# First batch of an attention and feed-forward kernel: tile 1's scores in two PSUM banks of their own, the order of all engines for tiles 0 to 3 rewritten, two weight pieces requested at once

## The chip, the cores and the metric

The kernel runs on one NeuronCore of one Trainium2 chip. The metric is the device time of one execution in microseconds (us), as the median of several runs. A NeuronCore has five engines that run their own instruction streams and meet at semaphores: TensorE (PE, matrix products), VectorE (DVE), ScalarE (ACT), GpSimd (POOL) and SyncE (SP), which here only starts transfers. Sixteen DMA engines move the data for all of them.

## The reference, cut to what matters

Three stages follow each other. Stage one is attention in chunks of 32 queries; each chunk sees its own keys, 16 before, 8 after, and 8 memory keys. Stages two and three are feed-forward layers on its output.

```python
# q, k, v: (batch 4, heads 8, seq 768, dim 64); mem_k, mem_v: (4, 8, 8, 64)
for c in range(seq // 32):
    k_full = concat(mem_k, k[c_start - 16 : c_end + 8])      # clipped at both ends
    scores = (q_c @ k_full.T) / 8
    a = exp(scores - max(scores)); a = a / (sum(a) + 1e-9)
    out[c] = a @ v_full
x = out as (3072 tokens, 512)
h = x @ w_in                                    # 512 x 1024
solu = h * softmax(h)
x2 = (layernorm(solu) * g_ln) @ w_out           # 1024 x 512
h2 = x2 @ w2_in; g = h2 * clip(h2 + 3, 0, 6) / 6     # 512 x 2048
result = g @ w2_out                             # 2048 x 512
```

## The kernel before, in words

The kernel is written engine by engine, in one block with a function for each engine, and the orders of the instructions are written out by hand. Nothing reorders them: an engine that waits holds back everything behind it in its own list.

Attention goes in tiles of 96 queries. A batch has 8 tiles with all 8 heads of 96 queries each, and there are 4 batches. A tile n passes through these helpers:

- SP loads `q_in`, `k_in` and `v_in` (`load_q`, `load_k`, `load_v`; two buffers of each, by the tile's parity). The sources have rows of 64 floats, so that they move in pieces of 256 bytes. A window of keys takes four transfers, and a fifth for the memory keys in tiles 0 and 1. `load_q(0, t)` waits until the query tile two before has been transposed, `load_k(0, t)` likewise for keys. All of these transfers leave on SP's queue (q1 in the rows); for tile 0 part of the keys leaves on ACT's (q10).
- PE transposes them into PSUM (`turn_q`, `turn_k`, L991), ACT copies them out (`copy_q`, `copy_k`), PE makes the scores (`scores`, L1044), in 48 small products.
- DVE takes the maximum of half the heads (`max_half`, L1786), ACT the exponentials of that half (`exp_half`, L1497), DVE the sum and its reciprocal (`den_half`, `rec_half`) and the scaling (`scale_half`, L1806).
- PE transposes the probabilities by halves (`turn_half`, L1052), ACT copies them (`copy_half`, L1472), PE makes the weighted sum of values (`attend`, L1073), and ACT and DVE split it into a high and a low part (`high_x`, `low_x`), which is the input x of the next stage.

In a call such as `exp_half(1, 0)` the first number is the tile and the second the half. Stage two works on 128 tokens at a time. `hidden_part(m, x)` (L1114) is a quarter of h for token block m, six products of 512 columns. Block 0 needs x of tiles 0 and 1 (`x_lo_done` 2), and of `w_in` it needs the split pieces 0 and 1 in part 0 and pieces 2 and 3 in part 1 (`w_lo_done` 2 and 4). After part 3 come `max_hidden`, `exp_hidden` (L1512), `solu_of` (L1853), the statistics, and the normalisation on POOL.

The weights come in eight pieces of 512 KB, four of `w_in` and four of `w_out`. POOL requests each (`load_weights`, on the software queue q0) and casts it to its high part (`high_weights`); DVE makes the low part of the first four (`low_weights`, L1771). The first request waits for the first query tile.

Only in the first batch is all of this written out (`first_batch` of each engine), because the pipeline fills there: PE has no products of stage two to do yet. `keep_busy(n)` gives PE n products of 128 by 128 whose result nobody reads. From the second batch on, a regular pattern (`batch`) runs with PE's products back to back. Tile n's scores are in PSUM banks 0 and 1, for every n, so that `scores(n)` waits for the exponentials of tile n-1.

Of the kernel before, what the change touches and what calls it, by code (L numbers as in the profile page):

```python
# [11 lines left out]
P = 128  # L12
# [6 lines left out]
def attention_solu_hardswish(  # L19
# [69 lines left out]
    with ExitStack() as ctx:  # L89
# [80 lines left out]
        score_ps = banks[0:TQ, 0:2, :].rearrange("p b (h n) -> p (b h) n", n=NK)  # L170
        turn_ps = [banks[:, 2, :], banks[:, 3, :]]
# [190 lines left out]

        def is_ahead(n):
            return n >= NA - AHEAD
# [94 lines left out]
        def _(sp):  # L459
# [228 lines left out]
        def _(pool):  # L688
# [60 lines left out]
            pool.wait_ge(fixed_ready, HALF_READY)  # L749
            pool.wait_ge(q_in_here[0], 16)  # L750

            def first_batch():
                load_weights(0)
                high_weights(0)
                load_weights(1)
# [3 lines left out]
                load_gain()  # L759
# [227 lines left out]
        def _(pe):  # L987
# [39 lines left out]
            def scores(n, very_first):  # L1027
# [7 lines left out]
                if very_first:  # L1035
                    pe.wait_ge(score_cleared, 2)
                else:
                    pe.wait_ge(sexp_done, 2 * n)
                for x in range(HB):
                    for c in range(TQ // CHUNK):  # L1040
                        rows = slice(CHUNK * c, CHUNK * (c + 1))
                        for e in range(2):
                            r = slice(D * e, D * e + D)
                            mm = pe.matmul(chunk_cols(score_ps[rows, HB * e + x, :], c), q_of[r, x, rows],  # L1044
# [126 lines left out]
            def keep_busy(times):  # L1171


                for _ in range(times):
                    pe.matmul(banks[:, 7, 0:P], ident[:, :], ident[:, :], start=True, stop=True)

            def first_batch():
                pe.wait_ge(fixed_ready, IDENT_READY)
                keep_busy(8)
# [4 lines left out]
                scores(0, True)  # L1184
# [12 lines left out]
                scores(2, False)  # L1197
# [3 lines left out]
                keep_busy(4)  # L1201
# [3 lines left out]
                keep_busy(2)  # L1205
                pe.wait_ge(prob_copied, 2)
                turn_half(1, 1)
                keep_busy(2)
# [21 lines left out]
                scores(4, False)  # L1230
# [15 lines left out]
                scores(5, False)  # L1246
# [25 lines left out]
                scores(6, False)  # L1272
# [21 lines left out]
                scores(7, False)  # L1294
# [11 lines left out]
            def batch(b, last=False, start=0):  # L1306
                for kk in range(start, TILES):
# [16 lines left out]
                    if w["own"]:  # L1324
                        scores(n, False)
# [113 lines left out]
        def _(act):  # L1439
# [50 lines left out]
            def exp_half(n, half):  # L1490
# [5 lines left out]
                for h in range(HB * half, HB * (half + 1)):  # L1496
                    last = nc.scalar.activation(prob[n % 2][:, h, :], score_ps[:, h, :], ACT.Exp, bias=smax[:, h:h + 1],  # L1497
# [70 lines left out]
            def first_batch():  # L1568
# [200 lines left out]
        def _(dve):  # L1769
# [3 lines left out]
            def clear_scores():  # L1773
                for half in range(2):
                    nc.vector.memset(score_ps[:, HB * half:HB * (half + 1), :], MASKED).then_inc(score_cleared, 1)

            def max_half(n, half):
# [8 lines left out]
                nc.vector.tensor_reduce(smax[:, hs], score_ps[:, hs, :], AX_X, ALU.max, negate=True  # L1786
# [121 lines left out]
            def first_batch():  # L1908
# [4 lines left out]
                max_half(1, 0)  # L1913
                den_half(0, 1)
                scale_half(0, 0)
                rec_half(0, 1)
                max_half(1, 1)
                scale_half(0, 1)
                den_half(1, 0)
                rec_half(1, 0)  # L1920
                low_weights(0)
                scale_half(1, 0)
                den_half(1, 1)
                rec_half(1, 1)
                max_half(2, 0)
                scale_half(1, 1)
                low_weights(1)
                max_half(2, 1)
                low_x(0, 0, 0)
                den_half(2, 0)  # L1930
                rec_half(2, 0)
                low_weights(2)
                scale_half(2, 0)
                low_x(1, 1, 0)
                low_weights(3)
                den_half(2, 1)
                max_half(3, 0)
                rec_half(2, 1)
                scale_half(2, 1)
                max_half(3, 1)  # L1940
# [270 lines left out]
```

## Time and profile before

| | us |
|---|---|
| median of 3 runs | 904.52 (903.02 to 905.22) |
| the profiled execution's own time | 903.32 |
| its span, from the first instruction to the last | 901.5 |
| PE busy | 876.4 |
| DVE busy | 646.7 |
| ACT busy | 460.5 |
| POOL busy | 263.8 |

The span is what the profile's clock covers, and the execution's own time holds 1.8 us around it. Engines overlap, so that busy times don't add up. All of the change lies in about the first 40 us of the span.

### The profile page before, as it was taken

To read this page: it belongs to the slowest core of one execution; us is meant where nothing else is said; L and a number is where in the kernel's file an instruction comes from. 1 tells how busy PE (TensorE), PEld (TensorE's weight loads), DVE (VectorE), ACT (ScalarE), POOL (GpSimd) and SP (SyncE) were. 2 spreads that over 40 slices of the span, in tenths; PEclk is the share of its full clock that TensorE was granted. 3 is DMA by queue.
4 is the path that set the end of the run, shared out by engine and by line. 5 is a ranking of instruction groups with operands and counts; after the bars stand their busy time and mean duration, and the time that the engine had idled before them with its cause. 6 is when DMAs were issued, how large, how long until landed. Compare 5 with 4: busy or idle time off the path is not lost.

```text
span 901.5 us, 18748 instructions
## 1 busy us (share of the span) xinstructions
PE 876.4 (97%) x7170; PEld 792.1 (88%) x7170; DVE 646.7 (72%) x1054; ACT 460.5 (51%) x1129; POOL 263.8 (29%) x308
## 2 busy tenths in 40 slices
PE   6899999999999999999999999999999999999998
PEld 5778988898888989899888888888799999999998
DVE  4768768787666778857685545554898887979784
ACT  5667555656565554537674555545754333333331
POOL 2474355465241453550122333223510000000000
PEclk8999999999999999999999999999999999999999
DMA  9965265554644474477733333333996434354341
GB/s 194 192 147 159 73 181 162 178 173 135 176 131 133 121 231 149 155 262 286 268 114 138 129 118 129 136 140 109 352 371 237 151 102 157 96 162 140 118 141 47
DMA packets 143496, 148.56 MB, mean 165 GB/s; under 512 B 91194, under 2 KB 102970, under 8 KB 142394
## 3 DMA queue, kind: packets, MB, share of 16 engines
q1 hardware_dynamic: 130272, 102.12, 37.3%
q0 software_dynamic: 7920, 38.94, 12.5%
q10 hardware_dynamic: 5226, 6.44, 2.2%
q8 instruction: 52, 0.85, 0.4%
q14 instruction: 26, 0.21, 0.1%
HBM read 89.92 MB, written 57.54 MB: 164 GB/s over the span
## 4 chain that ended last, share of the span: by engine, by line
PE 83%; DMA 5%; DVE 5%; ACT 3%; POOL 2%; issue 1%; SPq 1%; ACTq 0%; POOLq 0%; DVEq 0%
PE banks L1408 25%; PE banks L1147 25%; PE banks L1099 20%; PE banks L1114 3%; PE banks L1073 3%; PE banks L1044 2%; PE banks L991 2%; PE banks L1052 2%; PE banks L1090 2%; ACT prob L1497 1%; DMA xs_raw<-x_scratch 1%; POOL x_mix L897 1%; DMA x_mix<-x_scratch 1%; DMA x_mix_scratch<-x_mix 1%; DVE prob L1806 1%
## 5 line engine op out<-in xcount | busy, mean ns | idle before, releaser
L1408 PE MATMUL banks<-vs,gs 128*128 128x256 f32 x2016 | 242.8, 283 | 0.9 <-DMA vs<-v_split_scratch 0.8
L1408 PEld LDWEIGHTS banks<-vs,gs 128*128 128x128 f32 x2016 | 242.2, 192 | 1.6 <-DVE gs L1771 1.1
L1147 PE MATMUL banks<-xs,ws 128*128 128x512 f32 x1008 | 230.6, 390 | 0.5 <-ACT part L1550 0.2
L1147 PEld LDWEIGHTS banks<-xs,ws 128*128 128x128 f32 x1008 | 188.2, 188 | 41.6 <-issue 1.9
L1728 ACT CAST gs<-gs_raw 128x1792 fp32r<-128x1792 f32 x48 | 81.4, 1697 | 124.0 <-DVE gs_raw L2104 124.0
L1099 PE MATMUL banks<-y_t,w_out 128*128 128x384 f32 x768 | 141.1, 338 | 0.0
L1099 PEld LDWEIGHTS banks<-y_t,w_out 128*128 128x128 f32 x768 | 133.1, 188 | 0.8
L1099 PE MATMUL banks<-w_in,x_t 128*128 128x512 f32 x480 | 114.8, 395 | 1.1 <-DVE solu L1853 1.1
L1099 PEld LDWEIGHTS banks<-w_in,x_t 128*128 128x128 f32 x480 | 88.7, 188 | 19.9 <-DVE solu L1853 1.3
L2104 DVE TENSOR_TENSOR gs_raw<-gs_raw 128x256 f32<-128x256 f32 x192 | 82.2, 429 | 31.8 <-DMA gs_raw<-g_scratch 26.7
L1771 DVE TENSOR_TENSOR gs<-gs_raw,gs 128x1792 fp32r<-128x1792 f32 (+2 forms) x50 | 97.5, 1953 | 0.0
L1566 ACT ACTIVATE relu<-part,small 128x512 f32<-128x512 f32 x72 | 52.2, 724 | 86.1 <-DVE part L1895 86.0
L1497 ACT ACTIVATE prob<-banks,small 96x128 f32<-96x128 f32 x256 | 89.6, 370 | 9.3 <-DVE small L1786 9.3
L1904 DVE SCALAR_TENSOR_TENSOR part<-relu,part 128x512 f32<-128x512 f32 x72 | 53.7, 745 | 44.4 <-ACT relu L1566 44.4
L1895 DVE TENSOR_TENSOR part<-part,banks 128x512 f32<-128x512 f32 x72 | 49.4, 686 | 43.4 <-PE banks L1147 43.1
L1806 DVE TENSOR_TENSOR prob<-prob,small 96x512 f32<-96x512 f32 x64 | 56.3, 879 | 1.9
L941 POOL TENSOR_TENSOR ws<-ws_raw,ws 128x256 fp32r<-128x256 f32 x42 | 34.6, 835 | 74.1 <-ACT ws L1529 74.1
L1472 ACT COPY prob_t<-banks 128x384 f32<-128x384 f32 x64 | 28.3, 482 | 53.3 <-PE banks L1052 49.4
L1497 ACT ACTIVATION_READ_ACCUMULATOR prob<-banks,small 96x1 f32 x256 | 53.6, 209 | 0.0
L1839 DVE TENSOR_REDUCE small<-banks 128x1 f32<-128x1024 f32 x24 | 29.3, 1221 | 26.2 <-PE banks L1099 18.0
L1550 ACT COPY part<-banks 128x512 f32<-128x512 f32 x72 | 41.7, 579 | 12.1 <-PE banks L1147 11.0
L1786 DVE TENSOR_REDUCE small<-banks 96x4 f32<-96x512 f32 x64 | 42.1, 681 | 7.6 <-PE banks L1044 6.4
(104 smaller groups left out, 1012.7 us busy)
## 6 DMA issues: line engine op xcount, KB each, us to landing
g_scratch<-part SPq DMA_DIRECT2D x96, 256.0 KB, 2.0
gs_raw<-g_scratch SPq DMA_DIRECT2D x45, 512.0 KB, 4.0
x_scratch<-x_out ACTq DMA_DIRECT2D x32, 192.0 KB, 3.8
out_dram<-o_stage SPq DMA_DIRECT2D x11, 512.0 KB, 5.7
q_in<-in_q_dram SPq DMA_DIRECT2D x28, 192.0 KB, 3.0
v_split_scratch<-v_split POOLq DMA_DIRECT2D x3, 1792.0 KB, 7.6
ws<-w_split_scratch SPq DMA_DIRECT2D x21, 256.0 KB, 6.2
vs<-v_split_scratch SPq DMA_DIRECT2D x3, 1792.0 KB, 10.2
```

The source lines that it names most:

```text
L1099: mm = pe.matmul(psum, stationary(a, kc), moving(m, kc), start=(x == 0), stop=(x == len(passes) - 1))
L1147: mm = pe.matmul(ps, ws[:, W_OF[i], a, kc, :], xs[g][X_OF[i]][:, m, kc, :], start=(fresh and x == 0), stop=(x == len(passes) - 1), skip_gr ...
L1408: mm = pe.matmul(m_ps[i][:, s, :], gs[x][:, a, G_OF[i], s * P:(s + 1) * P], vs[p][:, m, V_OF[i], :], start=(p == 0 and s == 0 and y == 0), ...
L1497: last = nc.scalar.activation(prob[n % 2][:, h, :], score_ps[:, h, :], ACT.Exp, bias=smax[:, h:h + 1], accum_out=ssum[:, h:h + 1])
L1566: nc.scalar.activation(relu[r][:, :], src, ACT.Relu, bias=three).then_inc(relu_done[kind], 1)
L1728: nc.scalar.copy(gs[n % NGS][:, HI, :, :], gs_raw[n % NGS][:, :, :]).then_inc(gs_hi_done, 1)
L1771: return nc.vector.tensor_tensor(dst, src, hi.bitcast(F32), ALU.subtract)
L1786: nc.vector.tensor_reduce(smax[:, hs], score_ps[:, hs, :], AX_X, ALU.max, negate=True).then_inc(smax_done, 1)
L1806: nc.vector.tensor_tensor(prob[n % 2][:, hs, :], prob[n % 2][:, hs, :], srec[:, hs].unsqueeze(2).broadcast_to([TQ, HB, NK]), ALU.mult).the ...
L1895: nc.vector.tensor_tensor(part[e][:, :], part[e][:, :], ps, ALU.add).then_inc(sum_done[kind], 1)
L1904: nc.vector.scalar_tensor_tensor(out=part[e][:, :], in0=relu[r][:, :], scalar=6.0, in1=acc_ps[g] if kind == 21 else part[e][:, :], op0=ALU ...
L2104: nc.vector.tensor_tensor(gs_raw[x][:, to, :], gs_raw[x][:, a, :], gs_raw[x][:, b, :], op).then_inc(gt_done, 1)
```

## The change

Tile 1's scores get PSUM banks 6 and 7 (`second_score_ps`), cleared at the start by two more memsets on DVE. `scores(1)` then waits for that clearing, and no longer for the exponentials of tile 0; `scores(2)` waits for tile 0's exponentials alone. The fillers of `keep_busy` write to other banks. POOL no longer waits for the first query tile, requests g_ln first and then weight pieces 0 and 1 one behind the other. SP requests the values of tiles 0 and 1 ahead of queries and keys of tile 3. The lists of PE, ACT and DVE are put in another order for tiles 0 to 3.

```diff
@@ SP, first_batch
                 load_k(0, 2)
+                load_v(0, 0)
+                load_v(0, 1)
                 load_q(0, 3)
                 load_k(0, 3)
-                load_v(0, 0)
-                load_v(0, 1)
                 load_q(0, 4)
@@ POOL
-            pool.wait_ge(fixed_ready, HALF_READY)
-            pool.wait_ge(q_in_here[0], 16)
             def first_batch():
+                load_gain()
                 load_weights(0)
+                load_weights(1)
                 high_weights(0)
-                load_weights(1)
                 load_weights(2)
                 high_weights(1)
                 load_weights(3)
-                load_gain()
                 high_weights(2)
@@ PE, scores
-                if very_first:
-                    pe.wait_ge(score_cleared, 2)
+                if n < 2:
+                    pe.wait_ge(score_cleared, 2 * n + 2)
                 else:
-                    pe.wait_ge(sexp_done, 2 * n)
+                    pe.wait_ge(sexp_done, 2 if n == 2 else 2 * n)
@@ PE, first_batch
                 pe.wait_ge(qk_copied, 2)
                 turn_k(1, early_ps[1])
-                keep_busy(4)
-                scores(1, False)
+                keep_busy(4, 3)
                 pe.wait_ge(qk_copied, 3)
                 turn_q(2, early_ps[0])
-                keep_busy(2)
+                scores(1)
                 pe.wait_ge(qk_copied, 4)
                 turn_k(2, early_ps[1])
+                keep_busy(6, 3)
                 turn_half(0, 0)
                 pe.wait_ge(qk_copied, 5)
                 turn_q(3, early_ps[0])
-                scores(2, False)
+                scores(2)
                 turn_half(0, 1)
                 pe.wait_ge(qk_copied, 6)
                 turn_k(3, early_ps[1])
-                keep_busy(4)
+                pe.wait_ge(sexp_done, 4)
+                keep_busy(4, 7)
                 pe.wait_ge(prob_copied, 1)
                 turn_half(1, 0)
                 attend(0, 0, True)
...
                 attend(0, 1, False)
-                keep_busy(3)
-                scores(3, False)
-                pe.wait_ge(prob_copied, 3)
-                turn_half(2, 0)
+                keep_busy(3, 7)
                 pe.wait_ge(qk_copied, 7)
                 hidden_part(0, 0)
                 hidden_part(0, 1)
+                pe.wait_ge(prob_copied, 3)
+                turn_half(2, 0)
                 pe.wait_ge(qk_copied, 8)
+                scores(3)
                 hidden_part(0, 2)
@@ ACT, first_batch
                 exp_half(0, 1)
+                act.wait_ge(scores_done, 4)
                 copy_q(2, early_ps)
                 copy_k(2, early_ps)
                 exp_half(1, 0)
+                copy_half(0, 0)
                 exp_half(1, 1)
-                copy_half(0, 0)
                 copy_half(0, 1)
                 act.wait_ge(scores_done, 6)
                 copy_q(3, early_ps)
                 act.wait_ge(av_done, 1)
                 copy_half(1, 0)
+                high_x(0, 0, 0)
                 copy_k(3, early_ps)
-                high_x(0, 0, 0)
+                copy_half(1, 1)
                 exp_half(2, 0)
-                copy_half(1, 1)
+                high_x(1, 1, 0)
                 exp_half(2, 1)
-                high_x(1, 1, 0)
                 copy_half(2, 0)
+                copy_half(2, 1)
                 exp_half(3, 0)
-                copy_half(2, 1)
```

SP's list, from `load_q(0, 3)` on, before. `q_in` is a query tile, `k_in` a window of keys in four transfers, `v_in` values; the six transfers of `v_in` are tile 0's.

```order
L475 DMA q_in<-in_q_dram 96x8x64
L422 DMA k_in<-in_k_dram 56x8x64
L422 DMA k_in<-in_k_dram 8x8x64
L422 DMA k_in<-in_k_dram 24x8x64
L422 DMA k_in<-in_k_dram 32x8x64
L422 DMA v_in<-in_v_dram 40x8x64
L422 DMA v_in<-in_v_dram 8x8x64
L422 DMA v_in<-in_v_dram 24x8x64
L422 DMA v_in<-in_v_dram 32x8x64
L426 DMA v_in<-in_mem_v_dram 8x8x64
L429 DMA v_in<-in_v_dram 16x8x64
```

SP's list of the change, from the last transfer of tile 0's values to the last of tile 3's keys.

```order
L433 DMA v_in<-in_v_dram 16x8x64
L426 DMA v_in<-in_v_dram 56x8x64
L426 DMA v_in<-in_v_dram 8x8x64
L426 DMA v_in<-in_v_dram 24x8x64
L426 DMA v_in<-in_v_dram 32x8x64
L430 DMA v_in<-in_mem_v_dram 8x8x64
L479 DMA q_in<-in_q_dram 96x8x64
L426 DMA k_in<-in_k_dram 56x8x64
L426 DMA k_in<-in_k_dram 8x8x64
L426 DMA k_in<-in_k_dram 24x8x64
L426 DMA k_in<-in_k_dram 32x8x64
```

Tile 3's queries and keys moved behind the eleven transfers of both value tiles; the last transfer of its keys stands where the last one of tile 1's values stood, the 30th of SP's list.

DVE's list before, from `low_weights(1)` to the first half of tile 2 scaled and after it. `w_in` rows are `low_weights`, `x_t` rows `low_x` of tiles 0 and 1, L1796 and L1801 `den_half` and `rec_half`.

```order
L1771 TENSOR_TENSOR w_in<-w_first,w_in 128x1024
L1786 TENSOR_REDUCE small<-banks 96x4
L1771 TENSOR_TENSOR x_t<-banks,x_t 128x4x96
L1796 TENSOR_SCALAR small<-small 96x4
L1801 RECIPROCAL small<-small 96x4
L1771 TENSOR_TENSOR w_in<-w_later,w_in 128x1024
L1806 TENSOR_TENSOR prob_60<-prob_60,small 96x512
L1771 TENSOR_TENSOR x_t<-banks,x_t 128x4x96
L1771 TENSOR_TENSOR w_in<-w_later,w_in 128x1024
```

DVE's list of the change over the same work.

```order
L1791 TENSOR_REDUCE small<-banks 96x4
L1775 TENSOR_TENSOR x_t<-banks,x_t 128x4x96
L1775 TENSOR_TENSOR w_in<-w_first,w_in 128x1024
L1775 TENSOR_TENSOR x_t<-banks,x_t 128x4x96
L1775 TENSOR_TENSOR w_in<-w_later,w_in 128x1024
L1801 TENSOR_SCALAR small<-small 96x4
L1806 RECIPROCAL small<-small 96x4
L1811 TENSOR_TENSOR prob_60<-prob_60,small 96x512
L1775 TENSOR_TENSOR w_in<-w_later,w_in 128x1024
```

The second `x_t` row (`low_x` of tile 1) moved ahead of `low_weights(2)` and of the scaling of tile 2, and `low_weights(1)` moved behind the first `x_t` row. Between the second `x_t` row and the last `w_in` row (`low_weights(3)`) there was nothing, and now there are four instructions.

## Rows read from the trace of the kernel before

**Rows 1.** The page: busy time, and the engines' shares of the last chain.

```profile
PE 876.4 (97%) x7170; PEld 792.1 (88%) x7170; DVE 646.7 (72%) x1054; ACT 460.5 (51%) x1129; POOL 263.8 (29%) x308
...
PE 83%; DMA 5%; DVE 5%; ACT 3%; POOL 2%; issue 1%; SPq 1%; ACTq 0%; POOLq 0%; DVEq 0%
```

**Rows 2.** Chain that ended last, first 43 us: start, us, what.

```profile
9.72 2.78 ACT prob L1497 x16
...
16.74 2.89 ACT prob L1497 x16
...
21.69 0.85 PE banks L991 x4
...
23.96 0.83 PE banks L1073 x16
...
26.05 1.51 ACT prob L1497 x8
...
29.76 0.67 PE banks L1044 x46
...
30.91 4.16 PE banks L1114 x18
...
38.11 1.21 ACT h_exp L1512 x2
```

**Rows 3.** Timeline of SP's queue: start, us, what was issued.

```profile
9.37 2.33 SPq L422 DMA_DIRECT2D k_in<-in_k_dram  x4
...
14.23 5.97 SPq L422 DMA_DIRECT2D v_in<-in_v_dram  x4
20.24 0.63 SPq L426 DMA_DIRECT2D v_in<-in_mem_v_dram  x1
20.92 0.32 SPq L475 DMA_DIRECT2D q_in<-in_q_dram  x1
24.25 0.32 SPq L497 DMA_DIRECT2D q_raw<-in_q_dram  x1
```

**Rows 4.** Tile q_in, 0 to 40 us: time from issue to landing.

```profile
DMA to landing us min/median/max: 3.0/4.9/5.9
```

**Rows 5.** Stretches: busy us (count) by engine, clock, DMA share, GB/s.

```profile
10.00:15.00 5.00, 2.37 (x55) 2.22 (x56) 1.78 (x6) 2.90 (x16) 2.05 (x3) 0.76 1.19 181
15.00:20.00 5.00, 2.12 (x30) 1.96 (x34) 3.14 (x8) 3.82 (x19) 2.42 (x3) 0.84 0.98 225
20.00:25.00 5.00, 5.00 (x86) 4.60 (x75) 4.47 (x7) 1.05 (x3) 2.08 (x2) 0.72 1.00 189
```

**Rows 6.** DMA queues, 10.74 to 22.35 us: packets, MB, share of 16 engines.

```profile
q1 hardware_dynamic: 3956, 0.96, 56.4%
q0 software_dynamic: 420, 1.49, 48.2%
```

**Rows 7.** Timeline of PE, ACT and DVE, to 48 us: start, us, instruction.

```profile
19.77 1.09 PE L1044 MATMUL banks<-k_t,q_t 64*32 64x64 f32 x48 [2.88 <-ACT prob L1497]
...
21.49 1.06 PE L991 MATMUL banks<-ident,k_in 128*128 128x128 f32 x4
...
24.82 0.48 ACT L1472 COPY prob_t<-banks 128x384 f32<-128x384 f32 x1 [2.22 <-PE banks L1073]
25.20 0.59 ACT L1447 COPY k_t<-banks 128x512 f32<-128x512 f32 x1
...
29.17 0.51 ACT L1507 CAST x_t<-banks 128x384 fp32r<-128x384 f32 x1
29.71 0.56 DVE L1771 TENSOR_TENSOR x_t<-banks,x_t 128x384 fp32r<-128x384 f32 x1
30.19 1.22 DVE L1771 TENSOR_TENSOR w_in<-w_later,w_in 128x1024 fp32r<-128x1024 f32 x1
...
40.23 1.27 DVE L1853 SCALAR_TENSOR_TENSOR solu<-h_exp,small,banks 128x1024 f32<-128x1024 f32 x1
...
47.66 0.60 PE L991 MATMUL banks<-ident,k_in 128*128 128x128 f32 x4
```

More of the change, by code:

```diff
@@ L170, in attention_solu_hardswish @@
         score_ps = banks[0:TQ, 0:2, :].rearrange("p b (h n) -> p (b h) n", n=NK)
+        second_score_ps = banks[0:TQ, 6:8, :].rearrange("p b (h n) -> p (b h) n", n=NK)
         turn_ps = [banks[:, 2, :], banks[:, 3, :]]
@@ L360, in attention_solu_hardswish, with scores_of @@
         IDENT_READY, THREE_READY, HALF_READY = 2, 3, 4
+        def scores_of(n):
+            return second_score_ps if n == 1 else score_ps
         def is_ahead(n):
@@ L1025, in turn_qk, with scores @@
                     turn(turn_ps[1], k_in[:, s], NK)
-            def scores(n, very_first):
+            def scores(n):
                 if is_ahead(n):
@@ L1043, in scores @@
                             r = slice(D * e, D * e + D)
-                            mm = pe.matmul(chunk_cols(score_ps[rows, HB * e + x, :], c), q_of[r, x, rows],
+                            mm = pe.matmul(chunk_cols(scores_of(n)[rows, HB * e + x, :], c), q_of[r, x, rows],
                                            chunk_cols(k_of[r, x, :], c), start=True, stop=True, skip_group_check=True)
@@ L1169, in begin_next, with keep_busy @@
                 product(i, 0, ps, fresh_bank)
-            def keep_busy(times):
+            def keep_busy(times, bank):
                 for _ in range(times):
-                    pe.matmul(banks[:, 7, 0:P], ident[:, :], ident[:, :], start=True, stop=True)
+                    pe.matmul(banks[:, bank, 0:P], ident[:, :], ident[:, :], start=True, stop=True)
             def first_batch():
                 pe.wait_ge(fixed_ready, IDENT_READY)
-                keep_busy(8)
+                keep_busy(8, 5)
                 turn_q(0, early_ps[0])
@@ L1183, in first_batch @@
                 turn_q(1, early_ps[0])
-                scores(0, True)
+                scores(0)
                 pe.wait_ge(qk_copied, 2)
                 turn_k(1, early_ps[1])
-                keep_busy(4)
-                scores(1, False)
+                keep_busy(4, 3)
                 pe.wait_ge(qk_copied, 3)
                 turn_q(2, early_ps[0])
-                keep_busy(2)
+                scores(1)
                 pe.wait_ge(qk_copied, 4)
                 turn_k(2, early_ps[1])
+                keep_busy(6, 3)
                 turn_half(0, 0)
@@ L1204, in first_batch @@
                 attend(0, 0, True)
[L1205 removed]
+                keep_busy(2, 7)
                 pe.wait_ge(prob_copied, 2)
                 turn_half(1, 1)
[L1208 removed]
+                keep_busy(2, 7)
                 attend(0, 1, False)
[L1210 to L1213 removed]
+                keep_busy(3, 7)
                 pe.wait_ge(qk_copied, 7)
@@ L1229, in first_batch @@
                 turn_half(3, 0)
-                scores(4, False)
+                scores(4)
                 pe.wait_ge(prob_copied, 7)
@@ L1245, in first_batch @@
                 attend(0, 3, False)
-                scores(5, False)
+                scores(5)
                 pe.wait_ge(qk_copied, 12)
@@ L1271, in first_batch @@
                 turn_half(5, 1)
-                scores(6, False)
+                scores(6)
                 attend(0, 5, False)
@@ L1293, in first_batch @@
                 turn_half(6, 1)
-                scores(7, False)
+                scores(7)
                 pe.wait_ge(ahead_copied, 7)
@@ L1324, in batch @@
                     if w["own"]:
-                        scores(n, False)
+                        scores(n)
                     if w["own"] and w["before"]:
@@ L1496, in exp_half @@
                 for h in range(HB * half, HB * (half + 1)):
-                    last = nc.scalar.activation(prob[n % 2][:, h, :], score_ps[:, h, :], ACT.Exp, bias=smax[:, h:h + 1],
+                    last = nc.scalar.activation(prob[n % 2][:, h, :], scores_of(n)[:, h, :], ACT.Exp, bias=smax[:, h:h + 1],
                                                 accum_out=ssum[:, h:h + 1])
@@ L1773, in clear_scores @@
             def clear_scores():
-                for half in range(2):
-                    nc.vector.memset(score_ps[:, HB * half:HB * (half + 1), :], MASKED).then_inc(score_cleared, 1)
+                for ps in (score_ps, second_score_ps):
+                    for half in range(2):
+                        nc.vector.memset(ps[:, HB * half:HB * (half + 1), :], MASKED).then_inc(score_cleared, 1)
             def max_half(n, half):
@@ L1913, in first_batch @@
                 max_half(1, 0)
+                scale_half(0, 0)
                 den_half(0, 1)
-                scale_half(0, 0)
                 rec_half(0, 1)
@@ L1918, in first_batch @@
                 scale_half(0, 1)
+                low_weights(0)
                 den_half(1, 0)
                 rec_half(1, 0)
-                low_weights(0)
                 scale_half(1, 0)
+                max_half(2, 0)
                 den_half(1, 1)
                 rec_half(1, 1)
-                max_half(2, 0)
                 scale_half(1, 1)
-                low_weights(1)
                 max_half(2, 1)
                 low_x(0, 0, 0)
+                low_weights(1)
+                low_x(1, 1, 0)
+                low_weights(2)
                 den_half(2, 0)
                 rec_half(2, 0)
-                low_weights(2)
                 scale_half(2, 0)
-                low_x(1, 1, 0)
                 low_weights(3)
                 den_half(2, 1)
-                max_half(3, 0)
                 rec_half(2, 1)
                 scale_half(2, 1)
+                max_half(3, 0)
                 max_half(3, 1)
```

2 lines of the change are left out of this document (1 added, 1 removed).

## The prediction

> **What bounds the kernel now.** First the page: PE is busy for 97% of the span and holds 83% of the chain that ended last [rows 1]. So from the second batch on, the kernel is a row of products, and a change of the first 40 us counts one for one where it moves the moment at which PE gets its products of stage two. The chain over the start shows what sets that moment [rows 2]: the exponentials of tile 0 at 9.72, those of tile 1 at 16.74, the transposition of tile 3's keys at 21.69, the attend of tile 0 at 23.96, half of tile 2's exponentials at 26.05, and only at 30.91 the products of `hidden_part(0, 0)`. Then `exp_hidden(0)` at 38.11 and `solu_of(0)` at 40.23 [rows 2, 7]. I take `solu_of(0)` as the mark: `hidden_part(1, 0)` waits for it, and all later blocks hang on one another in the same way in both kernels.
>
> The second thing to see is that the transfers are full. The stretches from 10 to 25 us show the DMA engines busy by 1.19, 0.98 and 1.00 of their time [rows 5]. From 10.74 to 22.35 us SP's queue took 56.4% of them and POOL's queue of weights 48.2%, together 105% [rows 6]. SP's timeline says the same: the four large transfers of tile 1's values took 5.97 us to hand over, against 2.33 us for the keys of tile 3, so SP was held by its own queue [rows 3].
>
> **The change, part by part.** The wait removed is real. `scores(1)` stood behind the exponentials of tile 0, and PE idled for it; the same wait before `scores(2)` is 2.88 us [rows 7]. But PE's new list still has `turn_q(3)` ahead of `scores(2)`, and `turn_k(3)` ahead of `turn_half(1, 0)` and of both attends. So the attends begin when the keys of tile 3 have landed. Call that time L.
>
> L before was early: handed over from 9.37 to 11.70 [rows 3]. Now eleven transfers of values stand ahead, and the last transfer of these keys has the place of the last one of tile 1's values, which was issued at 20.24. The query tile behind it was issued at 20.92 [rows 3]. A query tile took 3.0 us from issue to landing at the shortest and 5.9 at the longest [rows 4]. So L lies between 20.24 + 3.0 = 23.2 and 20.24 + 5.9 = 26.1. SP's queue has the same transfers up to that place as before, in another order. The weights ask for more: pieces 0 and 1 come 4 and 8 us sooner, so pieces 2 to 4 do too. A piece costs about 0.482 x 11.61 / (420 / 128) = 1.7 us of all engines [rows 6], and one piece more may fall before L; against it stands a queue that is never empty in the first 8 us. I take L = 24.9, between the two ends, and as outer bounds 21 (at the 225 GB/s of the best stretch, where the three together have a mean of 198 [rows 5], the 23 us up to L shrink to 20, and I leave one more for the landing) and 28 (nearly two pieces more ahead).
>
> The Trainium skill (DMA: Bandwidth & Descriptors, "Issuing engines are not separate DMA queues") says that transfers started by different engines run on the same 16 DMA engines and interleave, so that starting them together saves only the issuing time. By that rule asking for two pieces at once moves L by nothing or later, and L stays 24.9; if two pieces of 1.7 us fitted beside the queries for free, L would be 21.5. The 105% of before agree with the rule.
>
> From L to `low_x` of tile 1. PE: `turn_k(3)` 0.5 and four fillers of the same shape 0.5 (four 128x128 take 0.60 with the drain [rows 7]), `turn_half(1, 0)` 0.4, attend 0.9 [rows 2]: 2.3. ACT: `copy_half(1, 0)` 0.4, `high_x` 0.4, `copy_k(3)` 0.5, `copy_half(1, 1)` 0.4, half of tile 2's exponentials 1.4, `high_x` 0.5 (starts follow each other a tenth sooner than the durations say [rows 2, 7]): 3.6. In all 5.9, against 29.71 - 21.49 = 8.2 before [rows 7]. So here the new order gives 2.3 us. `low_x` of tile 1 starts at 24.9 + 5.9 = 30.8 (29.71 before).
>
> From there to `solu_of(0)`. Before, `low_weights(3)` came right behind `low_x` and ran from 30.19 [rows 7], so that PE had 18 products in one run (4.16 us [rows 2]). Now DVE has `low_x` 0.5, `low_weights(2)` 1.1, `den`, `rec` and `scale` of tile 2 1.05, `low_weights(3)` 1.2: `hidden_part(0, 1)`, which wants all four pieces, starts 3.9 us after `low_x` does. Then PE: six products 1.4, `turn_half(2, 0)` 0.3, `scores(3)` 0.7, six products 1.4, `turn_half(2, 1)` 0.3 and its way to ACT 0.1: 8.2 [rows 2]. ACT: `copy_half(2, 1)` 0.4, both halves of tile 3's exponentials 2.75, `copy_q(4)` 0.4, so `exp_hidden(0)` at 11.7. From `exp_hidden(0)` to `solu_of(0)` it was 40.23 - 38.11 = 2.1 [rows 2, 7], and DVE has the same work there. In all 13.8, against 40.23 - 29.71 = 10.5 before. The cause is that `scores(3)` and the copy ahead of tile 3's exponentials went behind products of stage two, and `exp_hidden(0)` is behind those exponentials on ACT. That costs 3.3 us, whatever L is.
>
> So `solu_of(0)` comes at 24.9 + 5.9 + 13.8 = 44.6: 4.4 us later. To this I add clock. TensorE was granted 0.72 to 0.84 of full speed in the three stretches in which it waited between products [rows 5], and `turn_k(3)` took 1.06 us there against 0.60 later [rows 7]: level 1.2 instead of 2.4 GHz. Now it will wait longest, up to tile 3's queries, just ahead of the 2.1 us of PE work behind L and the first hidden products. I take 1.0 us, with bounds 0 and 2. Sum: +5.4.
>
> At nothing I cost these. Two memsets on DVE, four instead of two: DVE idles until about 8 us. The first keys of tiles 0 and 1 delayed by two weight pieces: up to 3 us, but the exponentials of tile 1 would end by 22, ahead of L. `load_ahead_q(0)`, at 24.25 before [rows 3], waits for `low_weights(1)`, now behind `low_x` of tile 0 and so near 29.5, and with it tile 4's keys and tile 2's values; they are wanted at 41 and later, so their cover is the shift itself, and without that shift they would have 11 us left. The g_ln request: 4 KB. In the rest of the batch nothing is reordered, so no gap gives the 5 us back: I carry them whole.
>
> The profiled execution took 903.32 us, 1.2 below the median of 904.52. 903.32 + 5.4 = 908.7, and on the median 909.9.
>
> **The rivals.**
>
> *The transfers move faster than I think, and nothing changes.* With `turn_k(3)` at 21.49 + 2.3 - 3.3 = 20.5 us gains and losses cancel: L = 21 and no clock gives +0.5, so 905. For it: 225 GB/s were moved from 15 to 20 us and 181 from 10 to 15 [rows 5]; if the slow stretch is not a property of the small pieces, L comes sooner. Against it: 105% busy [rows 6].
>
> *Faster: the wait was the bound, and L isn't.* If the keys of tile 3 land by 16, the exponentials decide: tile 0's at 9.72 for 2.8, two copies 0.9, tile 1's with a copy between 3.2, so both tiles' exponentials are done by 16.6, where `turn_k(3)` has just been made. That is 5.4 us before 21.49; with 2.3 gained, 3.3 lost and 1.0 of clock, `solu_of(0)` comes 3.4 us sooner: 901. It decides from `turn_k(3)` before 17.8, 2.7 us ahead of the point where it cancels. For it: the chain names exponentials for 5.7 us of the first 20 [rows 2]. Against it: the queue's order.
>
> *Slower still.* L = 28, and the clock at 1.2 GHz all through: 28 - 24.9 = 3.1, and 1.0 more of clock, so +9.5: 914. For it: the weights take more than half of the engines where both queues have work.
>
> **How the numbers follow.** I give 0.54 to the forecast (+3 to +8, so 907.5 to 912.5), 0.20 to no change (902 to 907), 0.15 to faster (about 901) and 0.11 to slower still. A measurement of this kernel can tell 0.3%, 2.7 us, from no change. Predicted is 909.9. The range reaches over the upper part of no change and part of slower still: 903.5 to 913, leaving out faster and the far end. Slower by over 0.3% has all of the forecast and of slower still, 0.65; the same 0.20; faster 0.15.
>
> **What would show it.** Right: tile 3's queries and keys issued near 16 to 21 us and transposed near 23 and 25; PE idle ahead of `turn_q(3)` with the transfer as releaser; attend of tile 0 near 26.5; a gap of about 1.5 us between the first six and the next six hidden products, released by DVE's `low_weights(3)`; `exp_hidden(0)` near 42 to 44; the same distance between `solu_of(0)` and later blocks as before. Wrong: `turn_k(3)` before 21 us; or `hidden_part(0, 1)` right behind `hidden_part(0, 0)`; or a later idle time of PE that shrinks by what the start lost.

## The result

The changed kernel took 910.19 us as the median, against 903.14 for the kernel before, measured together: a ratio of 1.0076, interval 1.0054 to 1.0099. It is slower by 7.0 us. The median is that of six executions; one of them took 966.32 us at a granted clock of 0.847, it isn't in the ratio, and without it the median is 910.01. The forecast was 909.9 on a median before of 904.52. In profiled executions the span went from 901.5 to 908.2 us.

The page of the changed kernel: busy time, and the granted clock in tenths over 40 slices.

```profile
PE 876.7 (97%) x7178; PEld 791.6 (87%) x7178; DVE 647.3 (71%) x1056; ACT 459.5 (51%) x1129; POOL 261.1 (29%) x308
...
PEclk9899999999999999999999999999999999999999
```

PE's busy time is that of before within 0.3 us [rows 1]. Of the 6.7 us of span 6.4 are idle time of PE (31.5 us against 25.1). They come from the start: the mark of the prediction, `solu_of(0)`, is 8.7 us late, and 2 us of that are gone again by the end.

The chain that ended last, of the changed kernel, in its first 50 us: start, us, what.

```profile
17.53 7.61 DMA q_in<-in_q_dram
...
25.28 0.87 PE banks L993 x4
26.15 1.02 PE banks L1046 x48
...
28.00 0.98 PE banks L993 x4
...
30.36 0.83 PE banks L1075 x16
...
34.73 0.56 DVE x_t L1775
...
38.62 1.66 PE banks L1116 x6
...
43.64 2.89 ACT prob L1500 x16
...
46.90 1.09 ACT h_exp L1515 x2
```

Before, exponentials led to the attends [rows 2]. Now the chain goes from a transfer: tile 3's queries, issued at 17.53, and 7.61 us later they are there and PE transposes them. `scores(2)`, the keys, the fillers and the attend of tile 0 follow in PE's list.

The timeline of the changed kernel, rows of SP, then PE, then DVE: start, us, instruction; in brackets the idle time ahead and its releaser.

```profile
13.51 3.59 SPq L426 DMA_DIRECT2D v_in<-in_v_dram  x4
...
17.53 0.32 SPq L479 DMA_DIRECT2D q_in<-in_q_dram  x1
17.89 5.43 SPq L426 DMA_DIRECT2D k_in<-in_k_dram  x4
...
33.83 0.31 SPq L501 DMA_DIRECT2D q_raw<-in_q_dram  x1
...
12.59 1.09 PE L993 MATMUL banks<-ident,k_in 128*128 128x128 f32 x4 [4.15 <-DMA k_in<-in_mem_k_dram]
...
25.28 0.87 PE L993 MATMUL banks<-ident,q_in 96*128 96x96 f32 x4 [6.51 <-DMA q_in<-in_q_dram]
...
27.89 1.09 PE L993 MATMUL banks<-ident,k_in 128*128 128x128 f32 x4
...
35.39 1.62 PE L1116 MATMUL banks<-w_in,x_t 128*128 128x512 f32 x6 [0.59 <-issue]
38.62 1.66 PE L1116 MATMUL banks<-w_in,x_t 128*128 128x512 f32 x6 [1.61 <-DVE w_in L1775]
...
48.90 1.27 DVE L1858 SCALAR_TENSOR_TENSOR solu<-h_exp,small,banks 128x1024 f32<-128x1024 f32 x1
```

To be seen: SP held by its queue for 3.59 and 5.43 us; the keys of tile 1 transposed at 12.59 after 4.15 us of waiting (8.44 before); PE idle for 6.51 us until tile 3's queries at 25.28 (16.39 before); `turn_k(3)` at 27.89 (21.49 before [rows 7]); between the first and second six hidden products 1.61 us of waiting for DVE's `low_weights(3)`; and `solu_of(0)` at 48.90 (40.23 before [rows 7]). The numbers "before" without a group are from the same timeline of the kernel before. Its row of tile 1's keys:

```profile
8.44 0.66 PE L991 MATMUL banks<-ident,k_in 128*128 128x128 f32 x4
```

Two stretches of the changed kernel: busy us (count) of PE, its loads, DVE, ACT and POOL, then clock, DMA share, GB/s.

```profile
20.00:25.00 5.00, 0.00 (x0) 0.00 (x0) 2.25 (x5) 1.10 (x7) 1.04 (x1) 0.74 0.89 209
25.00:30.00 5.00, 4.72 (x70) 4.20 (x71) 2.65 (x5) 0.87 (x2) 2.40 (x3) 0.58 0.20 42
```

From 20 to 25 us PE makes nothing at all while the DMA engines are busy for 0.89 of the time; then they stand at 0.20, since SP's next transfer waits until 33.83 for `low_weights(1)` (24.25 before [rows 3]). PE's clock is 0.58 of full in the stretch in which it has work again, after it had stood idle from 18.8 to 25.3 us.

### The profile page after: what moved, and what is told of

It reads as the page before. It is cut to its first block, busy times and chain, and to the rows that moved or that the text cites. A ratio compares the mean times of both kernels' runs of the same rounds, so it can differ in the third digit from the quotient of the medians.

```text
span 908.2 us, 18766 instructions
## 1 busy us (share of the span) xinstructions
PE 876.7 (97%) x7178; PEld 791.6 (87%) x7178; DVE 647.3 (71%) x1056; ACT 459.5 (51%) x1129; POOL 261.1 (29%) x308
## 4 chain that ended last, share of the span: by engine, by line
PE 84%; DVE 7%; ACT 3%; DMA 3%; issue 1%; SPq 1%; DVEq 0%; ACTq 0%
PE banks L1411 25%; PE banks L1149 23%; PE banks L1101 23%; PE banks L1075 2%; PE banks L1116 2%; PE banks L1092 2%; PE banks L1046 2%; PE banks L993 2%; PE banks L1054 2%; DVE prob L1811 2%; DMA q_in<-in_q_dram 1%; ACT prob L1500 1%; DVE small L1801 1%; SPq L426 1%; DMA gs_raw<-g_scratch 1%
## 5 line engine op out<-in xcount | busy, mean ns | idle before, releaser
L1791 DVE TENSOR_REDUCE small<-banks 96x4 f32<-96x512 f32 x64 | 42.1, 682 | 11.7 <-PE banks L1046 10.5
L1844 DVE TENSOR_REDUCE small<-banks 128x1 f32<-128x1024 f32 x24 | 29.3, 1221 | 26.5 <-PE banks L1101 18.6
## 6 DMA issues: line engine op xcount, KB each, us to landing
vs<-v_split_scratch SPq DMA_DIRECT2D x3, 1792.0 KB, 10.4
```

Source lines behind the costliest of these rows:

```text
L1791: nc.vector.tensor_reduce(smax[:, hs], scores_of(n)[:, hs, :], AX_X, ALU.max, negate=True).then_inc(smax_done, 1)
```

## The experiments

All ratios are against the kernel before, run on the same chip; its medians in the three groups of runs were 902.4, 902.0 and 901.7 us. The first four experiments ran on one chip, the others on a second one. The changed kernel itself wasn't run again beside them. So a difference from its 910.19 us can also be taken from the two ratios, and both values are given where they differ.

### SP's order of before in the changed kernel

```diff
-                load_v(0, 0)
-                load_v(0, 1)
                 load_q(0, 3)
                 load_k(0, 3)
+                load_v(0, 0)
+                load_v(0, 1)
```

> The changed kernel with one thing undone: SP asks for queries and keys of tile 3 ahead of the values of tiles 0 and 1 again. Theory T (the place of tile 3's transfers behind the values is what holds PE until 25.3 us): tile 3's queries land near 16 us, the last of the four is now the values of tile 1, landing near 26, and only the attend of tile 1 waits for them; low_x of tile 1 starts near 28 instead of 34.7, and the time falls by 5 to 7 us, to 903 to 905. Rival O (the new order of PE, ACT and DVE is the loss, the transfers only fill its idle time): tile 3's queries land early, and the time stays within 1.5 us of 910.2.

904.85 us, ratio 1.0042 (1.0023 to 1.0061): of the 7 us an order of transfers alone gave back 5.3 by the medians and some 3 by the ratios. In its timeline PE's row is `turn_k(3)`, DVE's are `low_x` of tile 1 and `solu_of(0)`.

```profile
22.47 0.66 PE L993 MATMUL banks<-ident,k_in 128*128 128x128 f32 x4 [1.79 <-DMA k_in<-in_k_dram]
...
30.43 0.56 DVE L1775 TENSOR_TENSOR x_t<-banks,x_t 128x384 fp32r<-128x384 f32 x1 [0.92 <-ACT x_t L1510]
...
44.56 1.27 DVE L1858 SCALAR_TENSOR_TENSOR solu<-h_exp,small,banks 128x1024 f32<-128x1024 f32 x1
```

The keys of tile 3 come only at 22.5, after 1.79 us of waiting for their transfer (with POOL's start of before as well it is 18.4, see the version with both of before), and `low_x` of tile 1 at 30.4, not 28. The time is in the range that T gave; O is out.

### POOL's start of before in the changed kernel

```diff
+            pool.wait_ge(fixed_ready, HALF_READY)
+            pool.wait_ge(q_in_here[0], 16)
...
-                load_gain()
                 load_weights(0)
-                load_weights(1)
                 high_weights(0)
+                load_weights(1)
                 load_weights(2)
                 high_weights(1)
                 load_weights(3)
+                load_gain()
```

> The changed kernel with POOL's start undone: it waits for the first query tile, then asks for one weight piece at a time, g_ln later. T with the DMA engines full: one to one and a half weight pieces fewer (1.7 us each) move ahead of tile 3's queries, which land at 22 to 23.5 instead of 25.1, and the time falls by 2 to 3 us, to 907 to 908. O: no change. A third reading W (the weights did all of it, by starving the first keys): keys of tile 1 transposed at 8.5 instead of 12.6, and the time falls by 4 us or more.

907.63 us, ratio 1.0063 (1.0043 to 1.0083): 2.6 us came back by the medians, as T said, but only 1.2 by the ratios, and the two intervals overlap. `solu_of(0)` is 2.3 us sooner (46.63). PE's timeline: keys of tile 1, queries of tile 3, keys of tile 3.

```profile
8.63 0.63 PE L995 MATMUL banks<-ident,k_in 128*128 128x128 f32 x4 [0.33 <-DMA k_in<-in_mem_k_dram]
...
20.68 0.87 PE L995 MATMUL banks<-ident,q_in 96*128 96x96 f32 x4 [5.99 <-DMA q_in<-in_q_dram]
...
24.05 1.09 PE L995 MATMUL banks<-ident,k_in 128*128 128x128 f32 x4 [0.64 <-DMA k_in<-in_k_dram]
```

Tile 3's queries are there at 20.7 instead of 25.3, sooner than expected. The keys of tile 1 are back at 8.6 and yet PE waits 6 us for tile 3's queries: with the values ahead, the delay of the first keys is not what counts. `turn_k(3)` is 3.8 us sooner than in the changed kernel, `low_x` of tile 1 only 2.2 (32.51): between the two the same eight fillers took 1.92 us instead of 1.26 and the attend of tile 0 1.55 instead of 0.88.

### Both of before, with the new order of the other engines and the two banks

The edits of the two sections above together.

> Both undone: the transfers of before, with the new order of PE, ACT and DVE and the two banks of tile 1's scores. T: values of tile 1 land at 24.5, low_x of tile 1 starts near 26.5 against 29.7 before, and the 3.3 us that the new order costs behind it eat that: 902 to 904, no change from 903.1. O: slower than before by 3 us or more, since the order is all there.

902.55 us, ratio 1.0011 (0.9986 to 1.0035): no change. Beside the 907.63 us of the version above, which differs from this one by SP's order alone and ran on the same chip, it is the cleanest price of that order: 5.1 us (1.0063 against 1.0011). And the 904.85 us of the first one, which differs by POOL's start alone, give that start 2.3 us. Timeline: `scores(1)`, attend of tile 0; `low_x` of tile 1, `solu_of(0)`.

```profile
10.66 0.74 PE L1048 MATMUL banks<-k_t,q_t 64*32 64x64 f32 x48
...
21.41 0.88 PE L1077 MATMUL banks<-prob_t,v_in 128*64 128x96 f32 x16 [1.22 <-DMA v_in<-in_v_dram]
...
25.84 0.56 DVE L1777 TENSOR_TENSOR x_t<-banks,x_t 128x384 fp32r<-128x384 f32 x1 [0.93 <-ACT x_t L1512]
...
40.36 1.26 DVE L1860 SCALAR_TENSOR_TENSOR solu<-h_exp,small,banks 128x1024 f32<-128x1024 f32 x1
```

Here the order for tiles 0 to 3, with the two banks, is seen by itself. `low_x` of tile 1 comes 3.9 us sooner than before (29.71 [rows 7]); from it to `solu_of(0)` it takes 14.5 us instead of 10.5, and `solu_of(0)` is where it was. Both halves of the account are in one profile.

### SP's new order in the kernel before

```diff
+                load_v(0, 0)
+                load_v(0, 1)
                 load_q(0, 3)
                 load_k(0, 3)
-                load_v(0, 0)
-                load_v(0, 1)
```

> The kernel before with SP's new order alone. T: tile 3's queries land near 22.5 and its keys near 24.5, so turn_k(3) goes from 21.5 to 24.5 or 25, and the time rises by 2.5 to 4 us, to 906 to 907. O: within 1.5 us of 903.1.

906.24 us, ratio 1.0039 (1.0021 to 1.0058). The same edit costs where nothing else is changed. PE's row of tile 3's queries:

```profile
21.24 0.87 PE L991 MATMUL banks<-ident,q_in 96*128 96x96 f32 x4 [5.36 <-DMA q_in<-in_q_dram]
```

Its keys followed at 25.24, against 21.49 before [rows 7]: later than expected, and behind a wait for the transfer too.

### The order of before around the first hidden products

Transfers of before, with PE, ACT and DVE as follows (of DVE the first moves; `max_half(3, 0)` goes back ahead of `rec_half(2, 1)` too):

```diff
@@ PE
+                pe.wait_ge(qk_copied, 8)
+                scores(3)
+                pe.wait_ge(prob_copied, 3)
+                turn_half(2, 0)
                 hidden_part(0, 0)
                 hidden_part(0, 1)
-                pe.wait_ge(prob_copied, 3)
-                turn_half(2, 0)
-                pe.wait_ge(qk_copied, 8)
-                scores(3)
                 hidden_part(0, 2)
@@ ACT
                 copy_half(2, 0)
-                copy_half(2, 1)
                 exp_half(3, 0)
+                copy_half(2, 1)
                 exp_half(3, 1)
@@ DVE
                 low_weights(1)
-                low_x(1, 1, 0)
-                low_weights(2)
                 den_half(2, 0)
                 rec_half(2, 0)
+                low_weights(2)
                 scale_half(2, 0)
+                low_x(1, 1, 0)
                 low_weights(3)
```

> The transfers of before, the two banks and the new order up to the attends, but the order of before around the first hidden products: PE makes scores(3) and turn_half(2, 0) ahead of hidden_part(0, 0), ACT starts tile 3's exponentials ahead of copy_half(2, 1), and DVE has nothing between low_x of tile 1 and low_weights(3). T (the new order costs 3.3 us from low_x of tile 1 to solu_of(0), whatever the transfers do, and gains about as much ahead of it): low_x of tile 1 near 26.8, solu_of(0) near 37.8 against 40.2 before, the time 2 to 3 us below the kernel before, about 900. Rival S (that stretch is bound by something else, such as the exponentials of tile 3): solu_of(0) stays at 40, the time at 902 to 903.

899.96 us, ratio 0.9972 (0.9952 to 0.9993). The time is the expected one; the way there isn't. Timeline: attend of tile 1; `low_x` of tile 1, `solu_of(0)`.

```profile
26.86 1.55 PE L1077 MATMUL banks<-prob_t,v_in 128*64 128x96 f32 x16 [2.45 <-DMA v_in<-in_mem_v_dram]
...
28.96 0.56 DVE L1776 TENSOR_TENSOR x_t<-banks,x_t 128x384 fp32r<-128x384 f32 x1 [0.72 <-ACT x_t L1511]
...
40.97 1.27 DVE L1859 SCALAR_TENSOR_TENSOR solu<-h_exp,small,banks 128x1024 f32<-128x1024 f32 x1
```

`low_x` of tile 1 came at 29.0, since the values of tile 1 landed late (2.45 us of waiting), and `solu_of(0)` at 41.0, both later than expected. From one to the other it is 12.0 us, 2.5 less than in the version with both of before. The mark is 0.7 us behind that of the kernel before, and yet the median is 2 us under it. In the profiled executions 1.9 us of that lie further on: between two later `solu_of` the kernel before takes 24.57 us (109.28 to 133.85), with a stretch of low clock near 122 us, and this one 22.65 (below).

### The same in the changed kernel, transfers and all

> The changed kernel, transfers and all, with the order of before around the first hidden products alone. T: turn_k(3) stays near 28, and the 3.3 us that the new order costs behind low_x of tile 1 come back, less up to one for turning tile 2 first: 907 to 908. S: no change from 910.

907.70 us, ratio 1.0063 (1.0046 to 1.0079), in the expected range, 2.5 us below the changed kernel by the medians and 1.2 by the ratios, with intervals that overlap. DVE's rows, `low_x` of tile 1 and `solu_of(0)`:

```profile
37.16 0.55 DVE L1774 TENSOR_TENSOR x_t<-banks,x_t 128x384 fp32r<-128x384 f32 x1
...
47.54 1.27 DVE L1857 SCALAR_TENSOR_TENSOR solu<-h_exp,small,banks 128x1024 f32<-128x1024 f32 x1
```

The 10.4 us between them are those of before, and 3.8 less than in the changed kernel. But `low_x` itself is 2.4 later. DVE runs into it without a pause: its input is written at 34.99 to 35.49, and `low_weights(2)` and the scaling of tile 2, from 35.45 on, stand ahead of it again. So of this term some 1.4 us are net at the mark.

### A version against both

Transfers of before; then PE, ACT and DVE:

```diff
@@ PE
                 hidden_part(0, 0)
+                pe.wait_ge(qk_copied, 8)
+                scores(3)
                 hidden_part(0, 1)
                 pe.wait_ge(prob_copied, 3)
                 turn_half(2, 0)
-                pe.wait_ge(qk_copied, 8)
-                scores(3)
                 hidden_part(0, 2)
@@ ACT
-                copy_half(2, 0)
-                copy_half(2, 1)
                 exp_half(3, 0)
+                copy_half(2, 0)
                 exp_half(3, 1)
+                copy_half(2, 1)
@@ DVE
-                low_x(0, 0, 0)
                 low_weights(1)
-                low_x(1, 1, 0)
+                low_x(0, 0, 0)
                 low_weights(2)
+                low_x(1, 1, 0)
+                low_weights(3)
                 den_half(2, 0)
                 rec_half(2, 0)
                 scale_half(2, 0)
-                low_weights(3)
+                max_half(3, 0)
```

> A version that tries to be better than both: transfers of before; PE makes hidden_part(0, 0), then scores(3), then hidden_part(0, 1) and turn_half(2, 0); ACT copies tile 2's halves behind tile 3's exponentials, half by half; DVE puts low_weights(1) ahead of low_x of tile 0 into its idle time, low_weights(2) between the two low_x and low_weights(3) right behind. T: hidden products begin at 26.5, solu_of(0) near 37, the time 3 us below the kernel before, about 899.5. S: no gain over 902.

897.37 us, ratio 0.9940 (0.9916 to 0.9963), 2 us under what T said. The edit of DVE also takes `max_half(3, 0)` out of its old place further down. Its timeline: the first six hidden products, `scores(3)`, the next six without a gap; `low_x` of tile 1, `solu_of(0)`.

```profile
28.29 1.63 PE L1118 MATMUL banks<-w_in,x_t 128*128 128x512 f32 x6 [0.35 <-issue]
29.85 0.74 PE L1048 MATMUL banks<-k_t,q_t 64*32 64x64 f32 x48
30.52 1.66 PE L1118 MATMUL banks<-w_in,x_t 128*128 128x512 f32 x6
...
27.63 0.56 DVE L1777 TENSOR_TENSOR x_t<-banks,x_t 128x384 fp32r<-128x384 f32 x1 [2.00 <-ACT x_t L1512]
...
39.08 1.27 DVE L1860 SCALAR_TENSOR_TENSOR solu<-h_exp,small,banks 128x1024 f32<-128x1024 f32 x1
```

The gap is gone, and 11.4 us lie between the two marks. Both come later than expected, though: the hidden products at 28.3 instead of 26.5 and `solu_of(0)` at 39.1 instead of 37, 1.2 us before that of the kernel before. The better time isn't explained by the mark alone.

> The tuned version once more, on the same chip as the one with one bank: 897 to 898.5, 4 to 5 us under the kernel before.

899.57 us, ratio 0.9966 (0.9944 to 0.9988). Less than the first time and outside what I expected, but faster than the kernel before again. 2 to 5 us, 0.3 to 0.6% by the ratios, is what can be claimed. Its `low_x` of tile 1 and `solu_of(0)`:

```profile
28.28 0.56 DVE L1777 TENSOR_TENSOR x_t<-banks,x_t 128x384 fp32r<-128x384 f32 x1 [2.69 <-ACT x_t L1512]
...
40.73 1.27 DVE L1860 SCALAR_TENSOR_TENSOR solu<-h_exp,small,banks 128x1024 f32<-128x1024 f32 x1
```

These are two executions of one kernel, and `solu_of(0)` lies 1.65 us apart in them (39.08 and 40.73). Differences of 1 to 2 us between single profiled executions are no larger than that.

### One bank instead of two

The new order with the transfers of before, and the same in the version against both, with the edit below (and without the clearing of banks 6 and 7):

```diff
         def scores_of(n):
-            return second_score_ps if n == 1 else score_ps
+            return score_ps
@@ PE, scores
-                if n < 2:
-                    pe.wait_ge(score_cleared, 2 * n + 2)
+                if n < 1:
+                    pe.wait_ge(score_cleared, 2)
                 else:
-                    pe.wait_ge(sexp_done, 2 if n == 2 else 2 * n)
+                    pe.wait_ge(sexp_done, 2 * n)
```

> The transfers of before and the new order, but tile 1's scores in banks 0 and 1 as before, so that scores(1) waits for tile 0's exponentials. If the removed wait is worth nothing by itself (T: attend of tile 0 waits for the values of tile 0, which land at 21.3), the time is that of the version with two banks, 902 to 903.5. Rival B (the wait is what the early part gains from): tile 1's exponentials start 1.5 to 3 us later, and the time rises by as much, to 904 to 905.5.

906.06 us, ratio 1.0049 (1.0030 to 1.0068), against 902.55 with two banks on another chip: above even B's range. Its profiled execution, though, had a span of 900.4 us, below the one with two banks (901.0); it was the fastest of the twelve executions of its version, 902.22 us. Timeline: `scores(1)`; `low_x` of tile 1, `solu_of(0)`.

```profile
12.36 0.90 PE L1048 MATMUL banks<-k_t,q_t 64*32 64x64 f32 x48 [0.98 <-ACT prob L1502]
...
27.06 0.56 DVE L1777 TENSOR_TENSOR x_t<-banks,x_t 128x384 fp32r<-128x384 f32 x1 [0.34 <-ACT x_t L1512]
...
41.69 1.27 DVE L1860 SCALAR_TENSOR_TENSOR solu<-h_exp,small,banks 128x1024 f32<-128x1024 f32 x1
```

`scores(1)` comes 1.7 us later than with two banks, `low_x` 1.2 and `solu_of(0)` 1.3 later. The last two are within what one kernel shows from execution to execution.

> The tuned version with tile 1's scores in banks 0 and 1, waiting for tile 0's exponentials. If the banks' gain is real where the values of tiles 0 and 1 gate the attends (B, as the version with one bank and the new order suggested by 3.5 us in the medians but 1.3 us in the profiled runs): 899.5 to 901.5. If it is not (T: the values land later than tile 1's exponentials are ready either way): 897 to 898.5.

900.58 us, ratio 0.9997 (0.9974 to 1.0019), in B's range, against 899.57 with two banks on the same chip: 1 us, with intervals that overlap, and in the profiled executions `solu_of(0)` comes sooner with one bank (39.63 against 40.73). The banks are worth something between 1 and 3.5 us once the transfers don't cover them; the runs don't settle how much.

### POOL's new start in the kernel before

> The kernel before with POOL's new start alone: g_ln first, weight pieces 0 and 1 at once, no wait for the first query tile. In the changed kernel the keys of tile 1 were transposed at 12.6 instead of 8.4, and ACT's copy of them is ahead of tile 0's exponentials. F (this delay counts where the exponentials set the pace, as in the kernel before): tile 0's exponentials start near 14 instead of 9.7, low_x of tile 1 near 33, and the time rises by 2 to 4 us, to 904 to 906. G (my costing: the delay of the first keys is covered by something later): no change, 901 to 903.

907.50 us, ratio 1.0062 (1.0039 to 1.0086): 5.8 us, more than F had expected, and G is out. PE's rows, keys of tile 1 and `scores(1)`:

```profile
12.60 1.09 PE L989 MATMUL banks<-ident,k_in 128*128 128x128 f32 x4 [4.38 <-DMA k_in<-in_mem_k_dram]
...
17.22 1.10 PE L1042 MATMUL banks<-k_t,q_t 64*32 64x64 f32 x48 [1.83 <-ACT prob L1495]
```

The keys of tile 1 are transposed 4.2 us later, ACT's copy of them stands ahead of tile 0's exponentials, and `scores(1)` waits for those: 17.22 instead of 12.63. `solu_of(0)` is at 44.64, 4.4 us late. In the old order two weight pieces at the start delay the exponentials and all that hangs on them.

## Why the prediction was right, by its steps

**The transfers set the pace: right, and shown.** With POOL's start of before, the two orders of SP are 5.1 us apart on one chip (907.63 and 902.55); the same edit on the kernel before cost 3.9. The DMA engines were busy at 0.89 and more from 5 us on until tile 3's queries landed. The signs came in their order, but each late: queries and keys transposed at 25.28 and 27.89 (forecast 23 and 25), attend of tile 0 at 30.3 (26.5), `exp_hidden(0)` at 46.8 (42 to 44).

**L = 24.9: the size was off.** I let the keys decide. What PE waited for were the queries ahead of them, at 25.28, and `scores(2)` and `turn_half(0, 1)` came in between at half clock, so that `turn_k(3)` began at 27.89, 3.0 us after my L and close to the bound of 28. I had taken the work between the two as done while the keys were still on their way. The DMA engines are down to 0.10 of their time from 26 to 27 us, so the keys were there by about 26; the rest is this work of PE. The queries took 7.61 us from issue to landing, where I had 5.9 as the longest.

**From L to `low_x` of tile 1: 5.9 forecast and 1.0 for the clock on top, 6.84 measured** (27.89 to 34.73). The gain of the new order there is 1.4 us with the clock's loss in it. That the clock took just 1.0 is partly luck: with POOL's start of before the same stretch took 8.46 us (24.05 to 32.51). With the transfers of before, `low_x` is 3.9 us sooner.

**From there to `solu_of(0)`: 13.8 forecast, 14.2 measured, and 14.5 with the transfers of before.** That it holds whatever L is, is shown: the five profiles with the new order there have 14.1 to 14.6 us, the four with the order of before 10.4 to 10.7. With the order of before there, but the new one ahead of it and the transfers of before, it was 12.0. The predicted gap between the hidden products was 1.5, the measured one 1.61 us.

**Two requests at once: no gain, and "at nothing" was only half right.** Behind the values the delay of the first keys is covered. Still, POOL's start cost 1 to 3 us in the changed kernel, through tile 3's queries (25.28 instead of 20.68), and 5.8 in the old order. Its price belongs inside L: `turn_k(3)` is at 24.05 with the old start and at 27.89 with the new one. In L I had set one more weight piece against a queue that is never empty, and so had next to nothing for it; L was too early by that.

**The whole loss carried to the end: wrong, and it hid the error before.** `solu_of(0)` came 8.7 us late against 5.4 forecast. The end came 6.7 us late in the profiled executions. The chains of the two kernels show where it went, here that of the kernel before between 40 and 135 us (maximum of hidden blocks 2 and 3, then a run of products):

```profile
63.26 1.24 DVE small L1839
...
74.64 1.24 DVE small L1839
...
125.36 5.49 PE banks L1099 x24
```

and that of the changed kernel, the same three (the last is cut off by the end of the window at 135 us, hence 17 products):

```profile
70.84 1.24 DVE small L1844
...
82.24 1.24 DVE small L1844
...
131.12 3.89 PE banks L1101 x17
```

The distance is 7.6, 7.6 and 5.8 us. The first microsecond went by way of a stretch at half clock that fell on the products of hidden block 2 before and on others now. The next 1.8 lie between 100 and 130 us; the windows of that stretch, of the kernel before and of the changed one:

```profile
100.00:130.00 30.00, 28.52 (x272) 25.41 (x271) 22.34 (x39) 18.62 (x73) 14.19 (x16) 0.94 0.51 144
```

```profile
100.00:130.00 30.00, 28.84 (x350) 26.34 (x348) 24.11 (x43) 17.97 (x64) 15.59 (x17) 1.00 0.33 88
```

TensorE was granted 0.94 there before and 1.00 now, and 1.00 too in the stretch with the same work, 7.6 us later. That these clock losses moved or vanished is seen in one execution of each kernel. Whether it belongs to the change isn't shown: the 88 executions of the kernel before that ran beside the experiments differ as much among themselves, with a mean of 903.5 us for the 26 that were granted 0.992 over the whole span and of 898.6 for the 13 at 0.998. Of the distance, 5.9 us are left at 400 us, 5.5 at 433 and 6.6 where the last stage's products begin (654.32 and 660.89); why it grows again isn't known. So 909.9 against 910.19 is better than the steps behind it, and that is luck: 3.3 us too little at the mark, 2 us too much carried to the end, and a median before that was 903.14 when both were measured together and not 904.52, so that the difference forecast was 5.4 us and the one measured 7.0.

**The rivals.** That the waiting for exponentials was the bound holds only where the transfers are those of before; there the banks bring their 1 to 3.5 us. The rival in which gains and losses cancel is what the version with both of before shows (`turn_k(3)` at 18.36, 902.55 us), but the transfers of the change rule it out. "Slower still" didn't come in the time, though `turn_k(3)` at 27.89 was nearly its L of 28.

## What to carry to other kernels

Where DMA engines are full, an engine's list of requests is a schedule: count what stands ahead of each transfer in its queue, then look at which one the consumer's list asks for first, and at what stands between. A removed wait is worth nothing while a transfer ends later, and may be worth something once the transfer is moved (1 to 3.5 us here, not settled). And an order that brings one operand sooner can put work of as many microseconds behind it: compare two marks, one on each side.

## What the runs showed of the hardware

Two weight pieces of 512 KB requested in the first 4 us delayed the keys of tile 1, in pieces of 256 bytes on another queue, by 4.2 us (8.44 to 12.59), more than the 3.4 us that I had priced both pieces at; the kernel before with POOL's new start alone shows the same (12.60). And the granted clock differs where the instructions are the same: profiled executions of kernels that differ only in their first 40 us were granted 0.94 or 1.00 in the stretch from 100 to 130 us. One execution of each doesn't tell whether the kernel or the execution decides it, and executions of the kernel before alone ranged from 0.988 to 0.998 over the whole span.
